# Hand-over to the first tile: the keys of its first unit split by GpSimd, transposes inside the first up-product, values behind the first down-product

## The reference

```python
scores = scale * np.matmul(q_c, k_full.transpose(0, 1, 3, 2))
scores = scores - np.max(scores, axis=-1, keepdims=True)
a = np.exp(scores)
a = a / (np.sum(a, axis=-1, keepdims=True) + 1e-09)
out[:, :, c_start:c_end] = np.matmul(a, v_full)
...
h = x @ w_in                                        # 3072x512 @ 512x2048
g = np.maximum(h, 0.0) + alpha * np.minimum(h, 0.0)
y = g @ w_out                                       # 2048 -> 512
...
a = y @ w_a; b = y @ w_b                            # 512 -> 1536
return (a * b) @ w_out2                             # 1536 -> 512
```

## Time and profile before

| what | value |
|---|---|
| time, median of 3 runs | 1157.89 us (1156.91 to 1692.02) |
| the profiled execution, its own time | 1159.26 us |
| its span, first to last instruction | 1157.4 us |
| granted TensorE clock, mean | 1.000 |
| TensorE busy | 1146.9 us (99% of the span) |
| VectorE, ScalarE, GpSimd busy | 852.1, 658.7, 258.5 us |
| chain of work that ended last | TensorE 96%, VectorE 2%, ScalarE 1%, GpSimd 1% |

### The profile page before, as it was taken

One profiled execution on the slowest core, in us unless ns is written; L12 is line 12 of the kernel. 1 busy time (PEld: TensorE's weight loads), 2 busy tenths in 40 slices (PEclk: granted clock), 3 DMA queues, 4 the chain that ended last, 5 costly groups with the idle time before them and its releaser, 6 DMA issues.

```text
span 1157.4 us, 18782 instructions
## 1 busy us (share of the span) xinstructions
PE 1146.9 (99%) x6169; PEld 1046.7 (90%) x6171; DVE 852.1 (74%) x1910; ACT 658.7 (57%) x1539; POOL 258.5 (22%) x234
## 2 busy tenths in 40 slices
PE   8899999999999999999999999999999999999998
PEld 6899999999999999999999888888888888888887
DVE  6788777777777777777644589899466898566675
ACT  7887656556666666666434555565445565444453
POOL 4898333333333333333035000000000000000000
PEclk9999999999999999999999999999999999999999
DMA  7453212112112122120201564577412167312054
GB/s 292 133 168 101 90 62 89 61 61 88 63 59 92 60 91 65 61 96 28 74 29 37 193 216 147 211 261 255 164 37 73 37 200 262 138 37 73 1 179 167
DMA packets 35718, 131.72 MB, mean 114 GB/s; under 512 B 3456, under 2 KB 7936, under 8 KB 33344
## 3 DMA queue, kind: packets, MB, share of 16 engines
q1 hardware_dynamic: 34448, 129.16, 33.0%
q10 hardware_dynamic: 1200, 1.70, 0.4%
HBM read 107.26 MB, written 23.59 MB: 113 GB/s over the span
## 4 chain that ended last, share of the span: by engine, by line
PE 96%; DVE 2%; ACT 1%; POOL 1%; issue 0%; DMA 0%; DVEq 0%; POOLq 0%
PE bank L734 15%; PE bank L736 15%; PE bank L735 15%; PE bank L741 10%; PE bank L742 10%; PE bank L740 10%; PE pair_ps L741 5%; PE pair_ps L740 5%; PE pair_ps L742 5%; PE pair_ps L754 2%; PE pair_ps L811 2%; PE bank L785 2%; PE pair_ps L773 0%; DVE y_stage L1385 0%; DMA u_early<-units 0%
## 5 line engine op out<-in xcount | busy, mean ns | idle before, releaser
L1464 DVE SCALAR_TENSOR_TENSOR g_raw<-g_neg,al,bank 128x384 f32<-128x384 f32 x128 | 78.6, 614 | 109.1 <-ACT g_neg L1104 105.7
L1104 ACT ACTIVATE g_neg<-bank 128x384 f32<-128x384 f32 x128 | 63.1, 493 | 124.5 <-PE bank L736 124.0
L741 PE MATMUL bank<-yc,ws 128*128 128x512 f32 x324 | 126.0, 389 | 0.0
L740 PE MATMUL bank<-yc,ws 128*128 128x512 f32 x324 | 126.0, 389 | 0.0
L742 PE MATMUL bank<-yc,ws 128*128 128x512 f32 x324 | 126.0, 389 | 0.0
L1069 ACT ACTIVATE prob<-prob,neg_max 96x128 f32<-96x128 f32 x220 | 85.7, 391 | 66.9 <-DVE neg_max L1399 66.9
L659 POOL TENSOR_TENSOR v_parts<-u_raw,v_parts 128x256 fp32r<-128x256 f32 x53 | 44.9, 848 | 279.3 <-ACT v_parts L1041 279.3
L1263 ACT ACTIVATE p_split<-p_all 128x512 fp32r<-128x512 f32 x126 | 77.2, 630 | 52.9 <-PE bank L742 39.0
L1672 DVE TENSOR_TENSOR p_split<-p_all,p_split 128x512 fp32r<-128x512 f32 x126 | 85.0, 686 | 12.8 <-ACT p_split L1263 12.5
L734 PE MATMUL bank<-x_hi,w_first 128*128 (+1 forms) x256 | 86.7, 339 | 1.6 <-DVE x_lo L1452 0.8
L734 PE MATMUL bank<-x_hi,w_later 128*128 (+1 forms) x256 | 86.3, 337 | 0.0
(11 more groups left out here) (182 smaller groups left out, 3167.1 us busy)
## 6 DMA issues: line engine op xcount, KB each, us to landing
wo_parts<-wo_dram SPq DMA_DIRECT2D x42, 768.0 KB, 4.8
u_raw<-units SPq DMA_DIRECT2D x53, 576.0 KB, 3.7
wr<-w_ab SPq DMA_DIRECT2D x18, 1024.0 KB, 4.9
wo_dram<-wo_stage SPq DMA_DIRECT2D x14, 768.0 KB, 8.6
u_early<-units SPq DMA_DIRECT2D x10, 576.0 KB, 9.3
y_dram<-y_stage SPq DMA_DIRECT2D x6, 768.0 KB, 4.6
out<-o_stage SPq DMA_DIRECT2D x9, 512.0 KB, 4.6
y_stage<-w SPq DMA_DIRECT2D x16, 256.0 KB, 2.8
```

The source lines that it names most:

```text
L740: nc.tensor.matmul(out_ap, w_hi, m_hi, start=first, stop=False, skip_group_check=True)
L741: nc.tensor.matmul(out_ap, w_hi, m_lo, start=False, stop=False, skip_group_check=True)
L1104: nc.scalar.activation(g_neg[:, :], h_ps[:, 0:TOK], ACT.Relu, scale=-1.0).then_inc(neg_part, 1)
L1464: nc.vector.scalar_tensor_tensor(out=g_raw[:, :], in0=g_neg[:, :], scalar=al[:, j:j + 1], in1=h_ps[:, 0:TOK], op0=ALU.mult, op1=ALU.add).t ...
```

## The change

- ScalarE no longer splits the keys and queries of unit 9; GpSimd copies them to the high part itself (`hi_kq_first`), before its normalise(8), with a semaphore of its own. `lo_kq` counts one less for the later units.
- ScalarE's hi_kq(10) and hi_v(10) move from ahead of tile 0 into its step c = 0, behind hi_g(0). hi_v(8) goes ahead of hi_w(3), and hi_w(4) is taken ahead of the tile; so is GpSimd's lo_w(4), with lo_v(8) ahead of lo_w(3).
- In step c = 0 of tile 0 only: TensorE does the transposes of unit 8 inside up(0), ahead of its last step kt = 3; the two `keep_busy` matmuls there go; `mix` of unit 8 goes from inside up(1) to behind down(0).
- ScalarE in step c = 0: bend(0), split_pt(8), hi_g(0), hi_kq(10), hi_v(10), bend(1), exps(9), hi_g(1), split_x(8), hi_w(5), hi_kq(11), hi_v(11), hi_w(6), hi_w(7).
- VectorE in step c = 0: bend(0), split_pt(8), lo_g(0), softmax_max_parts(9), bend(1), normalise(9), sum_x(8), lo_g(1), split_x(8). The scaling of alpha goes ahead of the copy of the last early transposes.
- The loads on the sync queue keep their order (`w_loads` is the old `w_in_tile0`).

```diff
--- before.py
+++ after.py
@@ -192,6 +192,7 @@
 
 
         kq_hi_done = sem("kq_hi_done")
+        kq_first_done = sem("kq_first_done")
         q_lo_done = sem("q_lo_done")
         k_lo_done = sem("k_lo_done")
         v_hi_done = sem("v_hi_done")
@@ -335,9 +336,13 @@
         def w_in_prologue(u):
             return {0: (0,), 1: (1,), 3: (2,)}.get(u, ())
 
-        def w_in_tile0(j):
+        def w_loads(j):
             first = W_PROLOGUE + 2 * j
             return range(min(first, W1_UNITS), min(first + 2, W1_UNITS))
+
+        def w_in_tile0(j):
+
+            return w_loads(j)[1:] if j == 0 else w_loads(j)
 
         def products(n, k, mat):
 
@@ -501,8 +506,7 @@
                 if j % 2 == 0:
                     u = EARLY + 1 + j // 2
                     load_unit(u, u % 2)
-                for n in w_in_tile0(j):
-
+                for n in w_loads(j):
                     if n + W_STAGE + W_MORE < W1_UNITS:
                         load_w(n + W_STAGE + W_MORE)
             def store_y(t):
@@ -664,7 +668,10 @@
 
                 b, low = c % 2, slice(HEAD_DIM, P)
                 src = raw(u, b)
-                pool.wait_ge(kq_hi_done, kq_count(u))
+                if isinstance(u, int) and u == KQ_FIRST:
+                    pool.wait_ge(kq_first_done, 1)
+                else:
+                    pool.wait_ge(kq_hi_done, kq_count(u, 1))
                 nc.gpsimd.tensor_tensor(kq_hi[b][low, Q0:], src[low, Q0:V0], kq_hi[b][low, Q0:].bitcast(F32),
                                         ALU.subtract).then_inc(q_lo_done, 1)
                 pool.wait_ge(q_lo_done, kq_count(u))
@@ -688,14 +695,21 @@
                 pool.wait_ge(inv_done, u + 1)
                 nc.gpsimd.tensor_tensor(buf[:, :, :], buf[:, :, :], inverses(u % 2), ALU.mult).then_inc(prob_done, 1)
 
+            def hi_kq_first():
+                pool.wait_ge(early_loaded[KQ_FIRST], 16)
+                nc.gpsimd.tensor_copy(kq_hi[KQ_FIRST % 2], u_early[:, KQ_FIRST, 0:V0]).then_inc(kq_first_done, 1)
+
             for u in range(HEADS + 1):
+                if u == HEADS:
+                    hi_kq_first()
                 normalise(u)
                 for n in w_in_prologue(u):
                     lo_w(n)
             pool.wait_ge(prob_done, HEADS + 1)
             lo_kq(HEADS + 1, HEADS + 1)
+            lo_v(HEADS, HEADS)
             lo_w(W_PROLOGUE - 1)
-            lo_v(HEADS, HEADS)
+            lo_w(W_PROLOGUE)
             lo_v(HEADS + 1, HEADS + 1)
             for j in range(CH1):
                 if j % 2 == 0:
@@ -813,7 +827,7 @@
                                             pt_parts[:, c % 2, i].rearrange("p s q -> p (s q)"), start=True, stop=True)
                 last.then_inc(mixed, 1)
 
-            def up(t, j, x_at, first_tile, values=None):
+            def up(t, j, x_at, first_tile, values=None, probs=None):
 
                 n = t * CH1 + j
                 if not first_tile or j:
@@ -822,6 +836,8 @@
                     pe.wait_ge(w_lo_done, 2 * j + 1)
                 w = slot(2 * j)
                 for kt in range(KT):
+                    if probs and kt == KT - 1:
+                        transpose_probs(probs)
                     if j == 0:
 
                         pe.wait_ge(x_lo_done, t * HEADS + (2 * kt + 2))
@@ -856,19 +872,22 @@
                 x_at = pe.snap(parity(t) * (KT * TOK)) if not isinstance(t, int) else parity(t) * KT * TOK
                 for c in range(HEADS):
                     u = (t + 1) * HEADS + c
-                    up(t, 2 * c, x_at, first)
+                    start = first and c == 0
+                    up(t, 2 * c, x_at, first, None, u if start else None)
                     if attention:
-                        if first and c == 0:
-                            keep_busy(2)
-                        transpose_probs(u)
+                        if not start:
+                            transpose_probs(u)
                         if attention == 2 or c < HEADS - 1:
                             score(u + 1, (c + 1) % 2)
                     if c:
                         down(t, 2 * c - 1, first)
                     elif not first:
                         down(t - 1, CH1 - 1, False)
-                    up(t, 2 * c + 1, x_at, first, (u, c, attention == 2 or c < HEADS - 1) if attention else None)
+                    values = (u, c, attention == 2 or c < HEADS - 1) if attention else None
+                    up(t, 2 * c + 1, x_at, first, None if start else values)
                     down(t, 2 * c, first)
+                    if start:
+                        mix(*values)
 
 
             keep_busy(8)
@@ -1141,6 +1160,16 @@
                     bend(t, 2 * c, first)
                     split_pt(u, c % 2)
                     hi_g(t, 2 * c, first)
+                    if first and c == 0:
+                        hi_unit(u + 2, c + 2, 0)
+                        bend(t, 1, first)
+                        exps(u + 1, 1, prob, prob)
+                        hi_g(t, 1, first)
+                        split_x(u, c, x_at)
+                        weights(0)
+                        hi_unit(u + 3, c + 3, 1)
+                        weights(1)
+                        continue
                     weights(2 * c)
                     if c == 0 and not first:
                         empty_y(t - 1)
@@ -1160,14 +1189,12 @@
                 for n in w_in_prologue(u):
                     hi_w(n)
             split_x_early(PAIRS - 2, 1)
-            hi_kq(HEADS + 1, HEADS + 1, 0)
             split_x_early(PAIRS - 1, 0)
             split_x_early(PAIRS - 1, 1)
+            hi_v(HEADS, HEADS)
             hi_w(W_PROLOGUE - 1)
-            hi_v(HEADS, HEADS)
+            hi_w(W_PROLOGUE)
             hi_v(HEADS + 1, HEADS + 1)
-            hi_kq(HEADS + 2, HEADS + 2, 0)
-            hi_v(HEADS + 2, HEADS + 2)
             tile(0, 2)
             with act.Fori(1, TILES - 2) as t:
                 tile(t, 2)
@@ -1488,10 +1515,16 @@
                         split_pt(u, c % 2)
                     if first and c == 0:
                         lo_g(t, 0)
+                        softmax_max_parts(u + 1, 1, half)
+                        bend(t, 1, first)
+                        normalise(u + 1, 1)
+                        sum_x(u, c, x_at)
+                        lo_g(t, 1)
+                        split_x(u, c, x_at)
+                        continue
                     if more:
                         softmax_max_parts(u + 1, (c + 1) % 2, half if c < HEADS - 1 else half_after)
-                    if not (first and c == 0):
-                        lo_g(t, 2 * c)
+                    lo_g(t, 2 * c)
                     if c == 0 and not first:
                         empty_y(t - 1)
                     if attention:
@@ -1533,14 +1566,14 @@
                     copy_pt(u - 2)
                 if u >= 5:
                     split_x_early((u - 5) // 2, (u - 5) % 2)
+            dve.wait_ge(alpha_loaded, 16)
+            nc.vector.tensor_scalar(al[:, :], al[:, :], -1.0, 1.0, ALU.mult, ALU.add).then_inc(alpha_ready, 1)
             copy_pt(HEADS - 1)
             invert_sums(HEADS, 0)
             split_x_early(PAIRS - 2, 0)
             split_x_early(PAIRS - 2, 1)
             split_x_early(PAIRS - 1, 0)
             split_x_early(PAIRS - 1, 1)
-            dve.wait_ge(alpha_loaded, 16)
-            nc.vector.tensor_scalar(al[:, :], al[:, :], -1.0, 1.0, ALU.mult, ALU.add).then_inc(alpha_ready, 1)
             dve.wait_ge(alpha_ready, 1)
             tile(0, 2)
             for t in range(1, TILES - 2):
```

## The result

The changed kernel takes 1159.34 us (median of 11 runs, 1158.62 to 1161.73); the kernel before took 1157.52 in the runs beside it. The ratio is 1.0016, 95% interval 1.0008 to 1.0023: **1.8 us slower**, between 0.9 and 2.7, far within 2%. One of the 11 executions of before took 1692.02 us, for a reason that no trace shows; ratios are of the fast executions alone. The forecast was 1158.2 in a range of 1155.5 to 1160.0.

A forecast was written before the change was run, and what follows sets the result against it. TensorE, busy 1146.9 of 1157.4 us, was taken as the bound. The 3.4 us won at the hand-over were given back by mix(9) (+0.15), summing to +0.3 at up(4): 1157.89 + 0.3 = 1158.2 us, range 1155.5 to 1160.0.

The forecast's parts named there:

- the lead of the hand-over: Entering tile 0, stalls removed on TensorE let up(2) start at about 39.1 instead of 42.55, 3.4 us ahead.
- the signs named for being wrong: up(4) before 51.5, GpSimd copy over 2.9 us, TensorE waiting on GpSimd's weights, another long-cycle count, or clock under 1.
- the waits named for being right: TensorE idle about 1 us ahead of scores(10) or down(1), 1.9 ahead of up(3), 0.9 ahead of mix(9).
- First bend: ScalarE's first bend in tile 0 starts at 33.23 instead of 34.78, 1.55 us won.
- The step "VectorE's x_lo follow at once": VectorE's last four x_lo run from 30.97 to 32.45 without the 0.71 us of idle before them.
- neg_max of unit 9: VectorE in step c = 0: neg_max there at 37.2 instead of 38.76, so mix(8) no longer stalls 1.51 us.
- normalise(9): VectorE in step c = 0: sums, reciprocal and product take 1.08 to 1.75 us, the product 0.69 or, beside GpSimd, 1.36.
- x_summed and bend(2): Cycle 1: x_summed at 42.1, later than before; ScalarE's queued splits then put bend(2) at 45.5 against 44.83.
- mix(9), up(4): TensorE: mix(9) at 48.7 against 48.56, up(4) at 52.3 against 52.14, weight 8 from GpSimd just in time.
- Long cycles: Behind up(4): same schedule shifted, with the two cycles over 10 us kept; one less or more would be 0.8 us.
- The rival of the lead kept: bend(2) follows up(2) at once, so the hand-over's gain lasts: -3.4 us, 1154.5, or half, 1156.2; chance 0.12.
- The rival of the clock: TensorE's clock falls to half from 44.7 to up(4) at 52.3, costing 4.7 us: 1162.9; chance 0.05.

The follow-up runs named there:

- e1: Changed kernel with sum_x(8) put back ahead of normalise(9) on VectorE in step c = 0: 1157.63 us, ratio to before 1.0001.
- e2: Changed kernel with ScalarE's hi_w(5), hi_kq(11) and hi_v(11) moved ahead of split_x(8) in step c = 0: 1157.29 us, ratio to before 0.9999.
- e4: Changed kernel with the alpha scaling back at its old place, ahead of tile 0: 1158.56 us, ratio to before 1.0005.
- e10: Changed kernel with e2's move, alpha scaling back, and lo_w(4) held till lo_g(0) is done; sum_x(8) stays behind normalise(9): 1156.52 us, ratio to before 0.9991.
- e3: Changed kernel with the old order of values and sums in step c = 0, mix(8) back inside up(1): 1159.09 us, ratio to before 1.0013.
- e5: Changed kernel with one added wait on GpSimd, lo_w(4) starting only when lo_g(0) is done: 1158.02 us, ratio to before 1.0002.

## Why the prediction was right, and where its terms were off

The time lay in the range, and the mechanism of the forecast is the one found: the lead of the hand-over is real (2.9 us at up(2), forecast 3.4) and it is gone at mix(9), because x_summed comes behind normalise(9) and ScalarE's queue stands behind it. e1 and e2 show this. The sum came out at +0.3 at up(4), measured +1.04, and the median rose by 1.8: it is the wide range, not the sum, that holds the time, and two errors of the chain cancelled in part (below). Of the signs named for being wrong, one appeared, a wait of TensorE on GpSimd's weights (0.15 us); the waits named for being right were there, all smaller (0.63, 1.42 and 0.80 for about 1, 1.9 and 0.9). Term by term, from T7 (the forecast's times less 28.06):

- *First bend*: forecast 5.17, measured 5.60. The step "VectorE's x_lo follow at once" left out the alpha scaling, which the change moved onto the path. I had given it no price; it cost 0.28 (e4). For the rest, 0.15, the profile of e4 gives the place: ScalarE's last x_hi ahead of the bend start 2.15 after T7, behind an idle of 0.23 for TensorE's bank, where the forecast put them at 1.95 with no wait, and from there to the bend ScalarE does not idle.
- *neg_max of unit 9*: 9.1 forecast, 36.96 - 26.52 = 10.44 measured. lo_g(0) was taken at its 0.60 of before, though the change puts lo_w(4) beside it; it took 1.46. I applied the stretching by GpSimd to one of VectorE's instructions and not to the other.
- *normalise(9)*: I took 1.36 for its product, it was 0.69. lo_kq(10) ended at 39.15 when the product began at 39.08. This was luck: neg_max came 1.3 us late, and that carried the product past GpSimd's instruction. It hid about half of those 1.3.
- *x_summed and bend(2)*: 14.0 and 17.4 forecast, 14.73 and 17.88 measured. "bend(2) = x_summed + 3.4" was 3.15.
- *mix(9), up(4)*: 20.6 and 24.2 forecast, 21.16 and 25.12 measured. Weight 8, "just in time", was late by 0.15, and with the restarts from mix(9) to up(4) took 3.96 instead of 3.6.
- *Long cycles*: I forecast the same two. The changed kernel has two, but before has one or two, 0.7 us apart. 1.04 + 0.7 would fit the 1.8 between the medians and between the lower groups of runs (1158.6 and 1156.8). As an estimate, a short start of 26.5 and an end of 1128.7, plus the 1.75 by which the time exceeds the span in the changed kernel's profile, give 1156.9 for before. With no short start of before profiled, this is argued, not shown.

The rival of the lead kept is refuted for this order and true for another (e2, e10). The rival of the clock did not happen in the changed kernel's profile (1.00 throughout; one run of 11 had 0.998), and did in e3, with 2.5 us where I had put 4.7 (for a later and longer stretch).

## What to carry to other kernels

When a step is moved earlier, look at what its successor waits for on the *other* engines: here the values were put behind the first down-product and their sum behind a wait for the exponentials, and ScalarE, which takes its instructions in order, stood idle at that wait with five more behind it. Three of them were ready, and moving them ahead gave back more than the change had lost at up(4) (e2). Order a queue by when its inputs come, and put ready work ahead of the instruction that waits. And compare profiles from an event that both reach by the same instructions, when the difference is smaller than what the start of the kernel scatters.

## What the runs showed of the hardware that I had not expected

- A VectorE instruction with two operands in SBUF that starts while a GpSimd instruction runs is not slowed in proportion. It ends at a set time behind the end of that instruction: lo_g 0.42 us behind it (35.40 and 34.98 in the changed kernel, 34.96 and 34.54 in e4), the 96x512 product 0.55 (53.07 and 52.52 in before). So 0.56 us became 1.46. The alpha scaling, with one operand of 128x16, ended 0.02 behind the copy of the keys (27.36 and 27.34) and 0.03 behind GpSimd's instruction in before (33.50 and 33.47), so its 0.30 there was no undisturbed time either.
- It goes the other way where VectorE starts no later: lo_g at 53.69 in before took its 0.56, and GpSimd's instruction at 53.70 took 1.70 instead of 1.3. With GpSimd about 0.1 us ahead the rows show either: 0.55 us for lo_g at 47.45 and 1.55 for GpSimd's instruction at 47.32 in the changed kernel, 1.56 at 33.40 and 1.28 at 33.26 in e4. Holding GpSimd back by 0.84 us made the kernel 0.8 us faster by the profile (e5).
- GpSimd copies 128x896 floats in 0.93 us, as fast as ScalarE (0.95 in the earlier trace rows); its two-input instruction takes 1.3 for 128x512.
- A gap of 2.39 us in TensorE, 0.84 before it, brought the granted clock to half for some 7 us (e3). With gaps of 1.5 us it stayed at full in all profiles, but not in all runs: of the 33 runs of before beside e3, three had 0.999.
- The same kernel has one or two long cycles from run to run, for no difference in its first 24 us behind T7.
